# Attention, expert routing and feed-forward in one kernel: decay rows issued ahead of q and k, a second issuing queue, less zeroing, embeddings scaled later

## The reference

```python
# attention: B, H, S, D = 4, 8, 576, 64
scores = q @ k.T / sqrt(D)
cum = cumsum(log(clip(f, 1e-4, 1)), axis=-1)
scores = where(causal, -1e9, scores + cum[:, :, :, None] - cum[:, :, None, :])
attn = softmax(scores);  out = attn @ v
# routing to one of E = 8 experts: N = 2304 tokens, d = 512, F1 = 1024
xn, en = x / |x|, emb / |emb|
e = argmax(xn @ en.T / tau);  gate = softmax(...)[e]
y = gate * (relu(x @ w1[e]) @ w2[e])
# feed-forward, F2 = 2048
out = softplus(y @ w_in) @ w_out
```

## Time and profile before

| | |
|---|---|
| runs (three) | 1017.92, 1028.23, 1035.81 us; median 1028.23 |
| profiled execution, its own time | 1015.05 us |
| its span, first to last instruction | 1013.3 us |
| mean granted clock of TensorE | 0.974 |
| busy: TensorE matmul / VectorE / ScalarE / GpSimd | 947.2 / 540.6 / 406.0 / 327.7 us |

### The profile page before, as it was taken

The page is one execution under the profiler, slowest core; times in us unless marked ns, Lnnn a source line. Parts: engine busy times, 40 slices in busy tenths (PEclk is TensorE's granted clock), DMA queues, the critical chain, the costliest instruction groups (busy, mean ns, idle before and its releaser), DMA issues.

```text
span 1013.3 us, 17340 instructions
## 1 busy us (share of the span) xinstructions
PE 947.2 (93%) x5588; PEld 831.8 (82%) x5589; DVE 540.6 (53%) x1095; ACT 406.0 (40%) x684; POOL 327.7 (32%) x168
## 2 busy tenths in 40 slices
PE   3999999999962999999999989999999999999997
PEld 2788888899852777887888878989989999899896
DVE  8567767665555566566555555444344444444433
ACT  6465666678542111311222343333333333333332
POOL 7344443433657254543677541010010000100101
PEclk9899999999965999999999999999999999999999
DMA  5444545454187435462466610000010010000000
GB/s 130 91 102 93 114 88 113 93 131 120 49 294 233 140 123 167 157 209 90 157 219 220 212 52 22 11 32 21 11 42 21 11 41 10 31 0 0 32 1 31
DMA packets 53701, 94.17 MB, mean 93 GB/s; under 512 B 23392, under 2 KB 23392, under 8 KB 53152
## 3 DMA queue, kind: packets, MB, share of 16 engines
q1 hardware_dynamic: 36864, 46.47, 17.4%
q10 hardware_dynamic: 13888, 37.75, 11.3%
q0 software_dynamic: 2912, 9.46, 2.7%
HBM read 76.42 MB, written 17.22 MB: 92 GB/s over the span
## 4 chain that ended last, share of the span: by engine, by line
PE 85%; DVE 4%; issue 4%; POOL 3%; DMA 2%; SPq 1%; ACT 1%; DVEq 0%; POOLq 0%; ACTq 0%
PE ps L1381 19%; PE ps L1394 19%; PE ps L1338 11%; PE ps L1317 10%; PE ps L1171 8%; PE ps L1134 6%; PE ps L1157 4%; POOL xs_dram L513 2%; PE ps L1326 1%; PE ps L1204 1%; PE ps L1135 1%; DMA k<-cum_dram 1%; PE ps L1301 1%; PE ps L1191 1%; PE ps L1368 1%
## 5 line engine op out<-in xcount | busy, mean ns | idle before, releaser
L503 POOL TENSOR_TENSOR W<-raw,W 128x2048 fp32r<-128x2048 f32 x40 | 183.6, 4616 | 144.1 <-ACT W L681 135.2
L1394 PE MATMUL ps<-W,ghl 128*128 128x512 f32 x864 | 215.4, 394 | 1.3 <-DVE ghl L1066 1.3
L1381 PE MATMUL ps<-yTh,W 128*128 128x384 f32 x768 | 197.6, 338 | 2.0 <-DVE yTl L1054 2.0
L1394 PEld LDWEIGHTS ps<-W,ghl 128*128 128x128 f32 x864 | 160.4, 188 | 32.0 <-DVE ghl L1066 1.6
L1060 DVE SCALAR_TENSOR_TENSOR sp_a<-ps,sp_a 128x384 f32<-128x384 f32 x96 | 53.4, 557 | 208.5 <-ACT sp_a L710 208.5
L681 ACT CAST W<-raw 128x2048 fp32r<-128x2048 f32 x36 | 67.1, 1908 | 222.6 <-PE ps L1317 84.1
L706 ACT ACTIVATE sp_a<-ps 128x384 f32<-128x384 f32 x96 | 47.3, 492 | 257.1 <-PE ps L1381 253.2
L1381 PEld LDWEIGHTS ps<-yTh,W 128*128 128x128 f32 x768 | 139.9, 188 | 9.2 <-POOL W L503 2.2
L527 POOL DMA_INDIRECT out<-out_sb,out_row x18 | 17.3, 961 | 380.9 <-DVE out_sb L1079 379.1
L1381 PE MATMUL ps<-yTl,W 128*128 128x384 f32 x384 | 129.4, 337 | 0.0
L1171 PE MATMUL ps<-v_ring,pT_sb 128*128 128x100 f32 (+2 forms) x960 | 120.4, 267 | 1.8 <-DVE x_all L799 1.8
(11 more groups left out here) (187 smaller groups left out, 1263.3 us busy)
## 6 DMA issues: line engine op xcount, KB each, us to landing
raw<-w ACTq DMA_DIRECT2D x28, 1024.0 KB, 5.8
qk_raw<-qkT SPq DMA_DIRECT2D x64, 288.0 KB, 4.2
x_raw<-xs_dram SPq DMA_DIRECT2D x22, 257.0 KB, 3.9
ys_dram<-y_sb SPq DMA_DIRECT2D x21, 256.5 KB, 4.9
y_raw<-ys_dram SPq DMA_DIRECT2D x18, 256.5 KB, 2.6
v_ring<-v SPq DMA_DIRECT2D x32, 128.0 KB, 3.1
raw<-w SPq DMA_DIRECT2D x4, 1024.0 KB, 5.4
raw<-w_in ACTq DMA_DIRECT2D x4, 1024.0 KB, 5.0
```

Source lines behind the costliest of these rows:

```text
L503: pool.tensor_tensor(wcols(par, 1, c), RAW[c][:, :], wcols(par, 0, c).bitcast(F32), ALU.subtract).then_inc(wl_done, 1)
L1381: ins = pe.matmul(bank(f_ % 2, GN), W[:, a:a + P], y[par][:, c, :], start=(m == 0), stop=(m == 3 * DC - 1))
L1394: ins = pe.matmul(bank(2 + k), ghl[:, (f_ + 2) % 4, part, k * P:k * P + P], W[:, a:a + DM], start=(f_ == 0 and m == 0), stop=(f_ == FC2 - ...
```

## The change

- The decay of head h (from 3 on) is issued ahead of q and k of head h+2; that of head 2 ahead of the first v.
- The four DMAs of the decay rows of head 1 are issued by ScalarE, between `high_k(0)` and `high_k(1)`, behind waits for `cum_ready`, `rows_set` and `q2_ones`.
- VectorE zeroes 65 columns of the upper 64 partitions of PSUM in place of 1536 columns of all.
- That memset and the scaling of the embeddings come behind the maxima of head 0 and `high_q(2)`. TensorE's four transposes of the embeddings come behind `pe_step(1)` and VectorE's copy of them behind `dve_step(1)`.

```diff
             def load_head(h, s, more=True):
...
+                if late or h >= 3:
+                    sp.wait_ge(scores_ready, s_used)
+                    load_decay(h, s % 2)
                 if more:
                     sp.wait_ge(kl_done, h + 1)
                     sp.wait_ge(qh1_done, h + 1)
                     load_qk(h + 2, s % 2)
-                if late or h >= 2:
-                    sp.wait_ge(scores_ready, s_used)
-                if not late and h == 2:
-                    sp.wait_ge(cum_stored, 16)
-                load_decay(h, s % 2)
...
-            first_decay(0)
-            first_decay(1)
+            for part in range(2):
+                row = cum_hl[0:1, part, :].bitcast(F32)
+                sp.dma_start(q2[part:part + 1, 0, 0:S].bitcast(F32), row).then_inc(first_loaded[0], 16)
+                sp.dma_start(k2[2 + part:3 + part, 0, :].bitcast(F32), row).then_inc(first_loaded[0], 16)
             sp.dma_start(cum_dram, cum_hl[:, :, :].bitcast(F32)).then_inc(cum_stored, 16)
             for h in range(2):
                 sp.wait_ge(kl_done, h + 1)
                 sp.wait_ge(qh1_done, h + 1)
                 load_qk(h + 2, h)
+            sp.wait_ge(scores_ready, NU)
+            sp.wait_ge(cum_stored, 16)
+            load_decay(2, 0)
             sp.wait_ge(v_ones, 1)
...
             high_k(0, 0, 0)
+            act.wait_ge(cum_ready, 3)
+            act.wait_ge(rows_set, 1)
+            act.wait_ge(q2_ones, 1)
+            for part in range(2):
+                row = cum_hl[1:2, part, :].bitcast(F32)
+                act.dma_start(q2[part:part + 1, 1, 0:S].bitcast(F32), row).then_inc(first_loaded[1], 16)
+                act.dma_start(k2[2 + part:3 + part, 1, :].bitcast(F32), row).then_inc(first_loaded[1], 16)
             high_k(1, 1, 0)
...
-            nv.memset(ps[:, 4 * 512:7 * 512], 0.0).then_inc(psum_zeroed, 1)
-            dve.wait_ge(emb_act, 2)
...
+            def embeddings():
+                nv.memset(ps[64:P, 6 * 512 + (NB - 1) * VW:6 * 512 + NB * VW], 0.0).then_inc(psum_zeroed, 1)
+                dve.wait_ge(emb_act, 2)
...
             for h in range(2):
                 dve_step(h, h)
                 if h == 0:
+                    embeddings()
+                else:
                     dve.wait_ge(enT_in, 1)
                     nv.tensor_copy(enT[:, :, :], bank(7, DC * E).rearrange("p (c e) -> p c e", c=DC)).then_inc(enT_ready, 1)
...
             for h in range(2):
                 pe_step(h, h)
-                if h == 0:
+                if h == 1:
                     pe.wait_ge(emb_scaled, 3)
```

More of the change, by code:

```diff
@@ L311, in load_decay @@
                 sp.dma_start(k2[2:4, r, :].bitcast(F32), cum_dram[bass.ds(h, 1)].rearrange("o t s -> (o t) s")).then_inc(decay_loaded[r], 16)
[L313 to L318, removed]
             def load_v(h, r):
@@ L748, in _ @@
             high_q(1, 1, 0)
-            nv.memset(ps[:, 4 * 512:7 * 512], 0.0).then_inc(psum_zeroed, 1)
-            dve.wait_ge(emb_act, 2)
[L752 to L756, removed]
+            def embeddings():
+                nv.memset(ps[64:P, 6 * 512 + (NB - 1) * VW:6 * 512 + NB * VW], 0.0).then_inc(psum_zeroed, 1)
+                dve.wait_ge(emb_act, 2)
+                nv.tensor_scalar(emb_s[:, 2:3], emb_s[:, 1:2], 1e-6, None, ALU.add).then_inc(emb_scaled, 1)
+                dve.wait_ge(emb_scaled, 1)
+                nv.reciprocal(emb_s[:, 3:4], emb_s[:, 2:3]).then_inc(emb_scaled, 1)
+                dve.wait_ge(emb_scaled, 2)
+                nv.tensor_scalar(emb_n[:, :], emb_in[:, :], emb_s[:, 3:4], None, ALU.mult).then_inc(emb_scaled, 1)
             def maxima(h, s, units):
```

## The result

| | before | changed | difference |
|---|---|---|---|
| first measurement, median (20 runs each) | 1035.62 us | 1027.70 us | -7.9 us; ratio 0.9874 [0.9826, 0.9922] |
| the profiled executions, span / own time | 1013.3 / 1015.05 us | 1009.4 / 1011.15 us | -3.9 us |
| measured again, beside the experiments, median | 1015.12 us (11 runs) | 1010.02 us (5 runs) | -5.1 us; ratio 0.9943 [0.9922, 0.9964] |

A forecast was written before the change was run, and what follows sets the result against it. TensorE, holding 85% of the chain, was taken as the bound. Gains of 4.3 us (stall), 2.4 (clock) and 0.9 (later decay waits) sum to 7.6, taking the median from 1028.23 to 1020.6 us, range 1008 to 1033.

The forecast's parts named there:

- The bound and the stall: Setup: TensorE bounds; without its 5.13 us idle gap, scores of head 2 begin at 23.5, not 27.82: 4.3 us.
- The cover that the prediction named: Setup, SP: decay of head 2 issued about 16.5 and 17.0, landing by 20.6; v loads moved back 0.65 us harmlessly.
- The clock term: TensorE's work from the scores of head 2: at full clock 7.38 us, not 9.75 after idling; gain 2.4 us.
- The later waits: TensorE, heads 3 to 8: the two smaller waits for decay rows go, gain 0.9 us.
- ScalarE's queue: Setup: four issues move off SP, giving it 2.5 us; second `high_k` ready at 11.9, no cost on the path.
- Rival A: Setup: SP and ScalarE queues hold each other back, first scores up to 2.2 us late; time 1023; chance 0.10.
- The embeddings' place: Setup: maxima of head 1 start 0.4 us late, and four transposes add 0.41 us to TensorE's path.
- The sum at turn 8: TensorE's work starting at the scores of head 8 begins at 67.8, not 75.38: 7.6 us.
- B: Early heads: the wait moves to q, k or v transfers, 2 to 3 us late; gain 5, time 1023; chance 0.09.
- C: Expert phase: further meetings of VectorE's scaling with GpSimd cost 1.7 us each; with seven, time 1033; chance 0.12.
- D: Setup: reordering does not bite, SP reaches the decay of head 2 late; time 1027; chance 0.03.
- its bounds: Whole gain: 8.4 us without the embeddings' cost, 5.2 with the work of head 2 still at slow clock.

The follow-up runs named there:

- e1: Kernel before with only the decay rows issued early (head 2 ahead of the first v, later heads ahead of q and k), all on SP: 1009.92 us, 0.9945.
- e7: Kernel before with 80 matmuls of 128 columns keeping TensorE busy in the stall before the scores of head 2: 1017.59 us, one run, beside 1015.35.
- e9: e8 plus 50 small matmuls on TensorE before the first scores: 1007.72 us, ratio to the kernel before 0.9919.
- e6: Kernel before with only heads from 3 on reordered (decay ahead of q and k), head 2 as before: 1015.18 us, one run, beside 1015.35.
- e5: Kernel before with only the decay of head 2 issued ahead of the first v, later heads in old order: 1010.62 us, one run, beside 1015.35.
- e2: Kernel before with only the four decay-row issues of head 1 moved from SP to ScalarE: 1014.55 us, 0.9986.
- e4: e1 and e2 together on the kernel before, embeddings and memset in their old place: 1008.11 us, 0.9932.
- e10: e8 plus 76 small matmuls on TensorE, reaching up to the first scores: 1007.31 us, ratio to the kernel before 0.9920.
- e11: Changed kernel plus the same 76 matmuls as e10 before the first scores: 1007.05 us, ratio to the kernel before 0.9923.
- e3: Kernel before with only the smaller memset and the embeddings moved behind the maxima of head 0, their transposes behind `pe_step(1)`: 1016.91 us, 1.0017.
- e8: e4 with the small memset where the large one stood, embeddings in their old place: 1010.22 us, ratio to the kernel before 0.9940.

## Why the prediction was right, point by point

**The bound and the stall: right.** The decay order is the gain. Alone (e1) it has 7.1 of the 7.2 to 7.9 us at turn 8, and 5.7 us in the medians, where the whole change has 5.1. The first stall goes: turn 2 at 23.16 and 23.79, forecast 23.5. The cover that the prediction named held: decay issued at 16.41 and 16.70, no wait for it, and the v loads behind it hold nobody up.

**The clock term: right, and shown by e7.** Turn 2 takes 7.45 us and not 9.75 (forecast 7.38). A gap of 1.04 us before 21.80 left the rate full; e9's gap of 1.73 us before the first scores did not.

**The later waits: right in the sum, incomplete as a mechanism.** 0.9 us is what the loop's order costs while the long stall stands ahead of it (e6: 1.1). Without that stall it is 2.2 (e5), with head 3 as the next to be late. The changed kernel never shows it, as both orders change at once, so the sum was not touched.

**ScalarE's queue: right.** Four issues of 0.60 to 0.64 us, as SP's own 0.59, `high_k(1)` ready at 11.83 (forecast 11.9). One of SP's issues took 0.83 beside them. e2 gives 0.8 us at turn 8; on top of the decay order (e4) nothing is to be seen. Rival A had the first scores up to 2.2 us late; they started at 11.97 and 12.21 in place of 11.91, and in the later case SP's first issue of decay rows was 0.24 us later already, so that isn't the queues' doing.

**The embeddings' place: a cost, as said, and its size near where the multiply meets GpSimd.** Forecast 0.4 + 0.41 us. The maxima of head 1 started 0.2 us late, not 0.35, and the four transposes 0.4 us; with the clock equal (e10, e11), 0.35 to 0.44 remain, since turn 2 would otherwise have waited for k. Another pair with nearly the same clock, up at about 16 us in both, is the changed kernel's first profile and e9: 1.1 us at turn 2 and 0.8 at turn 8. The multiply took 1.14 us beside GpSimd's low part of q and ended 0.27 us behind it in the changed kernel; in e11, where it began 0.1 us ahead of GpSimd, it took 0.47. That is the contention that the prediction took from the earlier meeting and the Trainium skill's GPSIMD Engine Reference, section 8; the measurement agrees. So this part of the change brings nothing by itself (e3: 1.0017).

**The sum at turn 8: 7.6 forecast, 7.86 and 7.22 in the two profiles.**

**Rivals.** B did not come: no wait for `v_ring` or `qk_raw` in turns 2 to 4. C did not come as it was told: the meetings of VectorE's scaling with GpSimd repeat, three waits for `hTl` of 5.2 us in all between 340 and 610 us, in both profiles of the changed kernel as before. But its idea, that an earlier start shifts something in the expert phase, came in small: the fourth wait of 0.96 us in the second profile, behind a late load of x. D did not come.

**The step that failed** is one sentence: "All behind it follows TensorE or hangs on its ends, to the last instruction, so the span falls from 1013.3 to 1005.7." It fell to 1009.4 and 1008.3. The lead of 7.2 to 7.9 us at turn 8 is not handed on whole, and the profiles show three places. One is the end of the scatters in the first profile: the single wait of 3.17 us, and a late landing. The second is the expert phase, where 0.2 to 2.2 us go between the first x transposes and the last phase, 0.7 to 1.0 of them the fourth wait for `hTl` in the three profiles that have one; for the rest no cause is shown. The third recurs: in six of the 14 profiles the clock stands at half for some microseconds as the last phase begins. The table has the lead over before in each place, and the time from the start of the last phase to the end, which is 423.0 us before:

| | at turn 8 | at the first x transposes | at the last phase | at the end | last phase to end | window with a low clock |
|---|---|---|---|---|---|---|
| changed, first profile | 7.86 | 4.38 | 3.95 | 3.9 | 423.0 | none |
| changed, again | 7.22 | 7.68 | 6.71 | 5.0 | 424.7 | 0.70 (585 to 590) |
| e1 | 7.08 | 6.72 | 5.96 | 4.4 | 424.6 | 0.73 (585 to 590) |
| e2 | 0.77 | 1.06 | 0.50 | -0.9 | 424.4 | 0.72 (590 to 595) |
| e4 | 6.75 | 6.58 | 5.56 | 3.9 | 424.7 | 0.67 (585 to 590) |
| e7 | 2.50 | 1.21 | -0.97 | -2.5 | 424.5 | 0.74 (590 to 595) |
| e8 | 7.04 | 6.40 | 5.72 | 4.2 | 424.5 | 0.73 (585 to 590) |
| e9 | 8.62 | 8.13 | 6.78 | 6.7 | 423.1 | none |
| e10 | 9.50 | 8.58 | 8.12 | 8.1 | 423.0 | none |
| e11 | 9.06 | 9.97 | 8.31 | 8.3 | 423.0 | none |

Where the clock stays up, in e3, e5 and e6 too, the lead at the last phase is kept to 0.1 us over 423 us; where it falls, 1.4 to 1.7 us go. e2 and e7 have the decay of head 2 as late as before, so the early decay isn't needed for the fall; since the profile of before has none, a lead at the end beside a fall is too small by that much. That the forecast's 7.6 us agree with the 7.9 between the medians of the first measurement is therefore partly luck: measured again the gain is 5.1, a little under the smallest that its bounds allowed (5.2). The total of 1020.6 stood 7.1 us below the measured 1027.7 because the median of before was 1035.6 there and not 1028.2.

**Still open:** what decides whether the clock rises at 16, 18 or 21 us. The changed kernel did both of the first two. But all four kernels with the late rise (e1, e4, e5, e8) have the decay of head 2 early and the embeddings in their old place, and all five with the decay late rose at 16, although TensorE does the same work until 16 us in both, within 0.1 us; with one profile each, neither chance nor the program is ruled out. Open are also what decides whether the clock falls near 585; what the wait of 3.17 us was for; where e3 loses its 1.3 us; and why turn 2 takes 7.8 us and not 7.4 in e1, e4, e8 and e9 (0.20 us of it is a gap before the first product with v in that turn).

## What to carry to other kernels

When a small late transfer sits behind bulk ones on an in-order queue, issue it first, and price the idle engine's slow restart with it: turn 2 came 4.0 to 4.7 us earlier, and the clock gave 2.4 more. Look then for the same order in the loop behind it, since a long stall hides what comes next (0.9 us turned into 2.2). And a lead won early is not the gain at the end: follow it from stage to stage in two executions before explaining either number.

## What the runs showed of the hardware

- TensorE's rate at the start differs between executions of nearly the same program: the pair of 512-column matmuls goes from 1.20 to 0.71 us at about 16, 18 or 21 us. The changed kernel's own two profiles have turn 2 at 23.16 and 23.79. With TensorE busy from 5.7 us until the scores it is at the full rate from the first one, and turn 8 comes 1.2 to 1.8 us earlier (e11 against the changed kernel's two profiles).
- At the start of the last phase the granted clock fell to a mean of 0.67 to 0.74 over five microseconds in six of 14 profiles, in kernels with and without the early decay, and cost 1.4 to 1.7 us.
- After 50 matmuls in 4.6 us, an idle gap of 1.73 us (e9) was followed by a granted clock of 0.50 from about 13 to 16 us; gaps of 1.0 us behind 20 us were not (the changed kernel, turn 2 in 7.45 us).
- One-row transfers from SBUF to SBUF take 0.60 to 0.64 us to issue on ScalarE's queue, and the two-row ones from DRAM 0.25 us on SP's. With both queues issuing at once, one of SP's issues took 0.83 us in place of 0.59, and the scores behind them started 0.06 us later (the changed kernel's first profile).
- A VectorE operation of 0.47 us (e11) took 1.14 when it started beside a GpSimd one that was under way, and ended 0.27 us after it (the changed kernel's first profile).
